# A fused retention and feed-forward kernel: turning the normalized rows of the last stage on VectorE and by transfers, with the up projection six blocks ahead

## What is computed

```python
def _moe2_ref(x, w_in, w_out, g_ln):            # x: 3072 x 512, w_in: 512 x 1024, w_out: 1024 x 512
    h = x @ w_in
    h_max = np.max(h, axis=-1, keepdims=True)
    e = np.exp(h - h_max)
    sm = e / (np.sum(e, axis=-1, keepdims=True) + 1e-09)
    solu = h * sm
    mu = np.mean(solu, axis=-1, keepdims=True)
    var = np.mean((solu - mu) ** 2, axis=-1, keepdims=True)
    ln = (solu - mu) / np.sqrt(var + 1e-06) * g_ln
    return (ln @ w_out).astype(np.float32)
```

## Time and profile before

| | us |
|---|---|
| median of three runs | 980.58 (980.35 to 981.1) |
| profiled execution | 983.99 |
| its span, first to last instruction | 982.2 |
| TensorE busy | 958.3 (98%) |
| VectorE busy | 616.8 (63%) |
| ScalarE busy | 548.3 (56%) |
| GpSimd busy | 135.5 (14%) |

### The profile page before, as it was taken

How to read it: one execution, slowest core, us unless ns; L and a number is a source line. 1 busy time by engine, 2 the same in 40 slices (tenths; PEclk the granted TensorE clock), 3 DMA queues, 4 the chain that set the end, 5 groups by cost and what they waited for, 6 DMA issues and landing times.

```text
span 982.2 us, 15207 instructions
## 1 busy us (share of the span) xinstructions
PE 958.3 (98%) x5494; PEld 849.6 (86%) x5494; DVE 616.8 (63%) x1054; ACT 548.3 (56%) x940; POOL 135.5 (14%) x170
## 2 busy tenths in 40 slices
PE   8879899999999999999999999999999999999998
PEld 4666787887899999999999999999888888888887
DVE  3777886777778653544678877677554444544442
ACT  3554645555465442433445555554687776667765
POOL 4313401102015510000151101010000000000000
PEclk9989999999999999999999999999999999999999
DMA  8747636536143513131553735521411111111100
GB/s 264 226 138 213 185 134 184 171 141 185 54 182 113 193 49 114 65 113 57 174 200 117 242 116 179 178 81 43 161 44 43 43 43 43 43 43 43 46 29 33
DMA packets 82320, 116.03 MB, mean 118 GB/s; under 512 B 7120, under 2 KB 62800, under 8 KB 82256
## 3 DMA queue, kind: packets, MB, share of 16 engines
q1 hardware_dynamic: 76800, 98.79, 30.6%
q0 software_dynamic: 4736, 15.73, 4.6%
q10 hardware_dynamic: 720, 0.66, 0.2%
HBM read 77.41 MB, written 37.75 MB: 117 GB/s over the span
## 4 chain that ended last, share of the span: by engine, by line
PE 83%; DVE 5%; issue 3%; DMA 3%; ACT 2%; POOL 2%; SPq 1%; DVEq 0%; ACTq 0%; POOLq 0%
PE psum L884 10%; PE psum L887 10%; PE psum L886 10%; PE psum L359 9%; PE psum L361 9%; PE psum L360 9%; PE psum L922 6%; PE psum L920 6%; PE psum L923 6%; PE psum L777 3%; PE psum L811 2%; PE psum L964 2%; PE psum L801 2%; PE psum L790 2%; DMA w_raw<-weights 1%
## 5 line engine op out<-in xcount | busy, mean ns | idle before, releaser
L884 PE MATMUL psum<-xo_hi,w_hi 128*128 128x384 f32 x560 | 195.3, 349 | 6.7 <-DVE psum L1494 2.6
L887 PE MATMUL psum<-xo_hi,w_lo 128*128 128x384 f32 x560 | 188.4, 336 | 0.0
L886 PE MATMUL psum<-xo_lo,w_hi 128*128 128x384 f32 x560 | 188.3, 336 | 0.0
L884 PEld LDWEIGHTS psum<-xo_hi,w_hi 128*128 128x128 f32 x560 | 105.9, 189 | 13.1 <-DVE xo_lo L1480 3.8
L886 PEld LDWEIGHTS psum<-xo_lo,w_hi 128*128 128x128 f32 x560 | 105.9, 189 | 0.8 <-issue 0.3
L1102 ACT ACTIVATE xo_hi<-b 128x768 fp32r<-128x768 f32 x84 | 70.6, 846 | 63.6 <-PE psum L923 51.9
L887 PEld LDWEIGHTS psum<-xo_hi,w_lo 128*128 128x128 f32 x560 | 105.7, 189 | 0.0
L1374 DVE TENSOR_TENSOR xo_lo<-b,xo_hi 128x768 fp32r<-128x768 f32 x84 | 80.0, 955 | 34.3 <-ACT xo_hi L1102 34.0
L359 PE MATMUL psum<-w_in_hi,x_hi 128*128 128x512 f32 x192 | 76.8, 400 | 0.3 <-ACT h_buf L1223 0.3
L361 PE MATMUL psum<-w_in_hi,x_lo 128*128 128x512 f32 x192 | 74.9, 390 | 0.0
L360 PE MATMUL psum<-w_in_lo,x_hi 128*128 128x512 f32 x192 | 74.9, 390 | 0.0
(11 more groups left out here) (128 smaller groups left out, 2065.8 us busy)
## 6 DMA issues: line engine op xcount, KB each, us to landing
act_dram<-act_buf SPq DMA_DIRECT2D x48, 384.0 KB, 2.4
b<-act_dram SPq DMA_DIRECT2D x48, 384.0 KB, 4.8
kq_buf<-k_t SPq DMA_DIRECT2D x32, 192.0 KB, 2.7
kq_buf<-q_t SPq DMA_DIRECT2D x64, 96.0 KB, 3.0
q_dec<-q_t SPq DMA_DIRECT2D x32, 192.0 KB, 2.5
w_raw<-weights POOLq DMA_DIRECT2D x12, 512.0 KB, 4.6
x_dram<-x_tile SPq DMA_DIRECT2D x4, 1536.0 KB, 6.0
x_tile<-x_dram SPq DMA_DIRECT2D x4, 1536.0 KB, 6.8
```

The lines of the kernel that those rows point to most:

```text
L884: pe.matmul(dst, hi[:, cols], xo_hi[:, i, kc, :], start=i in (P1, P7) and kc == 0, stop=False, skip_group_check=True)
L886: pe.matmul(dst, hi[:, cols], xo_lo[:, i, kc, :], start=False, stop=False, skip_group_check=True)
L887: mm = pe.matmul(dst, lo[:, cols], xo_hi[:, i, kc, :], start=False, stop=kc == HK - 1, skip_group_check=True)
```

## The change

It touches the last stage alone.

- The first tile keeps the way of before, turns on TensorE included. From block (1,0) on TensorE turns nothing. Instead ScalarE squares solu with the negative mean as bias (`square_solu`) and takes the root for two blocks at once (`deviation_of_pair`); VectorE inverts two at once (`invert_pair`), normalizes (`normalize`, mean and inverse deviation in one instruction), and turns the rows in 32x32 squares (`turn_blocks`) into a buffer z.
- SP then moves the squares to their partitions (`move_turned`): 16 transfers a tile, each from 32 partitions to 32 partitions, 512-byte runs, 128 KB, four for each quarter of the tile. They wait for the last `turn_blocks` of the tile.
- A block of the down projection is now 32 consecutive tokens out of each of the four blocks of the tile, so that its output rows lie in four runs. The output isn't scaled any more, since the rows are normalized already. `ln_high` and `ln_low` read SBUF instead of PSUM.
- TensorE runs the up projection six blocks ahead of the down projection instead of two: in the first tile each step has two up projections, then one per block, and for the last six blocks none.
- The loop on the device is gone: all tiles are written out. There is one order for tiles 1 to 5.

The diff, cut to what sets the order. The moves and the rows of an output, on SP:

```diff
+            def move_turned(t):
+                for i in range(PARTS):
+                    sp.wait_ge(z_ready, BLOCKS * t)
+                    sp.wait_ge(ln_lo_ready, 2 * (BLOCKS * (t - 1) + i + 1))
+                    for f in range(PARTS):
+                        sp.dma_start(ln_t[32 * f:32 * f + 32, i, :, :],
+                                     z_of(t)[32 * i:32 * i + 32, :, f, :, :].rearrange("p k j c -> p k (j c)")).then_inc(
+                                         ln_t_moved[i], DMA)
...
+                if t == 0:
+                    rows = out[n * P:(n + 1) * P, :]
+                else:
+                    rows = out[bass.ds(t * TC, TC), :].rearrange("(b i c) d -> i b c d", b=BLOCKS, i=PARTS)[j]
```

SP in tiles 1 to 5:

```diff
+                if t + 2 < C_TILES:
+                    load_pair(t + 2)
+                store_out(t - 1, 3)
+                for j in range(3):
+                    store_out(t, j)
+                if t + 1 < C_TILES:
+                    move_turned(t + 1)
```

TensorE in the first tile from its second block on, and in tiles 1 to 5:

```diff
+                    for j in range(1, BLOCKS):
+                        turn(0, j)
+                        both_up((2 * j + 2) // BLOCKS, (2 * j + 2) % BLOCKS)
+                        both_down2(0, j)
+                        both_up((2 * j + 3) // BLOCKS, (2 * j + 3) % BLOCKS)
+                    return
                 for j in range(BLOCKS):
...
+                    if run_up_of(t, j):
+                        both_up(*run_up_of(t, j))
+                    both_down2(t, j)
```

ScalarE in tiles 1 to 5:

```diff
+                    if j > 0:
+                        scale_out(t, j - 1)
+                    elif t > 1:
                         scale_out(t - 1, 3)
                     ln_high(t, j, 0)
                     ln_high(t, j, 1)
+                    last_up = (t + 1, j + 1) if j < 3 else (t + 2, 0)
+                    if last_up[0] < C_TILES:
+                        square_solu(*last_up)
+                        if j % 2 == 0:
+                            deviation_of_pair(t + 1, j // 2)
+                    if run_up_of(t, j):
+                        copy_h(*run_up_of(t, j), 0)
+                        if j % 2 == 1 and t + 2 < C_TILES:
+                            x2_high(t + 2, j // 2)
+                        copy_h(*run_up_of(t, j), 1)
+                        exponent(*run_up_of(t, j))
```

VectorE, the two new steps, and tiles 1 to 5:

```diff
+            def normalize(t, j):
+                dve.wait_ge(pair_rstd_ready, 2 * (t - 1) + j // 2 + 1)
+                dve.tensor_scalar(solu[:, j % 2, :], solu[:, j % 2, :], mean[:, j:j + 1], rstd[:, j:j + 1], ALU.add,
+                                  ALU.mult).then_inc(normalized, 1)
+            def turn_blocks(t, j):
...
+                dve.transpose(z_of(t)[:, :, :, j, :].rearrange("p k f c -> p (k f) c"),
+                              solu[:, j % 2, :].rearrange("p (b r) -> p b r", r=32)).then_inc(z_ready, 1)
...
+                    both_low(t, j)
+                    if t + 1 < C_TILES:
+                        if j % 2 == 0:
+                            invert_pair(t + 1, j // 2)
+                        turn_up(t + 1, j)
+                    if run_up_of(t, j):
+                        row_max(*run_up_of(t, j))
+                        if j % 2 == 1 and t + 2 < C_TILES:
+                            x2_low(t + 2, j // 2)
+                        take_up(*run_up_of(t, j))
```

More of the change, by code:

```diff
@@ L336, in x_bank, with tiles, run_up_of, solu_of @@
             return SUM if n == 1 else PX
-        def loop(eng, n, step):
-            step(0, True, False)
-            with eng.Fori(1, n - 1) as i:
-                step(i, False, False)
-            step(n - 1, False, True)
-        def tiles(eng, step):
-            loop(eng, C_TILES, step)
+        def tiles(step):
+            for t in range(C_TILES):
+                step(t)
+        def run_up_of(t, j):
+            tile, block = (t + 1, j + 2) if j < 2 else (t + 2, j - 2)
+            return (tile, block) if tile < C_TILES else None
+        def solu_of(t, j):
+            return solu_0[:, j, :] if t == 0 else solu[:, j % 2, :]
+        def z_of(t):
+            return z1 if t % 2 else z0
         def windows(attention_step, point):
@@ L1027, in _ @@
+            tiles(stage_c)
         @block.scalar
@@ L1570, in softmax_h @@
                 dve.wait_ge(sum_inverted, n + 1)
-                dve.scalar_tensor_tensor(out=solu[:, j % 2, :], in0=h_buf[:, j % 2, :], scalar=e_inv[:, one],
+                if n == 0:
+                    for s in range(4):
+                        dve.wait_ge(x2_stored[s], DMA * 2 * B)
+                dve.scalar_tensor_tensor(out=solu_of(t, j), in0=h_buf[:, j % 2, :], scalar=e_inv[:, one],
                                          in1=e_buf[:, j % 2, :], op0=ALU.mult, op1=ALU.mult,
```

313 lines of the change are left out of this document (209 added, 104 removed).

## The result

The changed kernel takes **993.32 us** (median of 4 runs, 992.76 to 994.5) against 980.84 of the kernel before beside it: ratio 1.0125, 95% interval 1.0107 to 1.0143. Measured a second time it was 992.09 against 981.84, ratio 1.0096 (1.0070 to 1.0122). So the change costs 12.5 us by the first pair of medians and 10.3 by the second. The forecast was 985.0 with a range to 992.0: the sign was right, and the time lies outside the range.

What follows compares the result with a forecast made beforehand. TensorE's own work was taken to bound the third stage. The terms -17.4 + 14.1 + 1.3 + 5.3 + 1.1 gave +4.4 us, from a median of 980.58 to 985.0, range 978.5 to 992.

Steps and rivals of the forecast that it cites:

- turns leave TensorE, 20 blocks: Third stage after the first tile: TensorE loses the turns, 0.87 us a block over 20 blocks, -17.4 us.
- hand-overs in the tail: Last six blocks: TensorE waits while ScalarE puts output ahead of the high halves, 2.35 us each, +14.1 us.
- moves at (5,0): Block (5,0) in the tail: its moves land later than the hand-overs alone would allow, +1.3 us (0 to 5).
- first tile: First tile of the third stage: TensorE waits 2.9 and 2.2 us, +5.3 us with the restarts.
- rival (d): Tail: the granted clock falls where TensorE idles 2.3 of every 7.8 us; 6 us more, 991; chance 0.05.
- last store: Kernel's end: store in four runs of 32 rows, +2.2 us if on four DMA engines, else 0; +1.1 taken.
- What bounds the kernel: Third stage: it lasts as long as TensorE's own work; work leaving its queue comes off the end unless somebody becomes late.
- Steady tiles: Tiles 1 to 3: ScalarE about 7.5 and VectorE 7.1 us a block fit under TensorE's 10.90; the moves stay hidden.
- The tail's waits: Last six blocks: TensorE waits about 2.2 us for the low half five or six times, output ahead of high half.
- rival (a): First tile: its hand-over costs nothing and the last store is as before; -2.0 us, 978.6; chance 0.13.
- (e): Last store: dealt to four DMA engines, 2.2 us instead of 1.1, 986.1 in all; chance 0.3.
- Profiled execution and median: Whole kernel: profiled execution 983.99 us, median of the runs 980.58; differences were taken to carry over, giving 985.0.

Runs made afterwards that it cites:

- e5: Changed kernel plus nine extra 512-column products on TensorE ahead of each of the last six down projections: 987.17 us, ratio 1.0057.
- e7: Changed kernel with e1's order, last square and deviation also before output, two of (5,0)'s moves on ScalarE's queue, last store in four from two queues: 978.25 us.
- e8: e9 plus 14 extra 512-column products on TensorE ahead of the down projection of (5,0): 975.86 us, ratio 0.9938.
- e9: e7 with all four moves for block (5,0) issued by SyncE again: 977.38 us, ratio 0.9951.
- e4: Changed kernel with e1's order, last store as four transfers of 32 rows, and e3's earlier inverse together: 978.9 us, ratio 0.9965.
- e1: Changed kernel with ScalarE making the two high halves before scaling the previous block's output in the last six blocks: 981.4 us, ratio 0.9984.
- e3: Changed kernel with VectorE inverting the deviation of (0,3) before the turns of (1,2) and (1,3) in the first tile: 993.05 us, ratio 1.0101.

## Why the prediction was right in its sign and wrong in its size

Its sum, term by term, from the two traces of the changed kernel:

| step | forecast | measured |
|---|---|---|
| turns leave TensorE, 20 blocks | -17.4 | -17.8 (20 x (11.77 - 10.88)) |
| hand-overs in the tail | +14.1 | +13.4 (6 x 2.23) |
| moves at (5,0) | +1.3 | 0, hidden behind the half clock of (4,3); 1.1 in e5 |
| first tile | +5.3 | +4.7 to +4.9, what is left over of the chain |
| clock in the tail, rival (d) | 0 | +4.8 and +6.4 (3 and 4 stretches of 1.6) |
| last store | +1.1 | +3.8 |
| sum | +4.4 | +8.9 and +10.7 |

**What bounds the kernel: right.** TensorE's steady block fell to its 48 matmuls, and the 12 blocks between (1,1) and (4,1) took 130.56 us in nine of the twelve traces of this order. In e7, e8 and e9 it is 132.9, since there the output of (4,1) itself stands 2.4 us further back in ScalarE's queue; the eleven steps ahead of it are 10.88 as well.

**Steady tiles: right.** The 32x32 turn takes 1.246 us (1.2 forecast), normalization 0.81 (0.75), and VectorE 32.08 of 50 us, 7.0 a block (7.1). ScalarE was 7.0 (7.5). Sixteen moves are issued in 11 to 12 us (10) and in the steady tiles TensorE doesn't wait for them; the first quarter takes 5.8 us from its first issue to the start of the high half (e4), where I had 4.8 to its landing.

**The tail's waits: right** in place, number, releaser and size. e1 shows that the order of output and high half makes them.

**The first tile: near in its sum.** The two waits were forecast as 2.9 and 2.2 and are 2.3 and 1.5; in one trace the clock stood in for the second. The +4.7 to +4.9 is a remainder; the waits by themselves are 3.8 where 5.1 were forecast. e3 shows that the inverse behind the turns, which I held against rival (a), isn't the cause.

**The clock: the step that failed.** I weighed rival (d) with the slices of the page, in which TensorE is busy eight tenths at a clock of nine. A slice is 24.6 us long and says nothing of a stretch of 3 us behind a gap of 2. I also read slices one, two and five and passed over the third, the one nearest to the tail's share: TensorE is busy seven tenths there and the clock is at eight. The row that spoke for it, 0.83 in a window of 10 us with 8.40 us busy, was the nearest row by length, and the tail (5.8 of 8 us busy) lay below it. I gave the mechanism 6 us, near the 4.8 and 6.4 that it cost, but a chance of 0.05 and nothing in the sum. e5 settles the cause: fill the gap and it is gone.

**The last store: a term mis-sized.** The mechanism of (e) was right, and its price was 3.8 us, beyond my upper end of 2.2. The end counted the data at a quarter of the rate (3.0 us; the trace has 256 KB at up to 103 GB/s) and left out the 2 us at under 50 GB/s ahead of it. I also took the middle of two ends where a stated rule pointed to one.

**Profiled execution and median.** I carried the differences from an execution of 983.99 us over to a median of 980.58. The part ahead of the change varies by 3.5 us between executions (716.9 to 720.4), so the sum holds against a chain of the stage, not against one execution's time; this added up to 3.5 us of uncertainty that the range didn't have. It bears on the miss: with the chains' +8.9 and +10.7 on 980.58 the time would have been 989.5 and 991.3, inside the range with the clock and the store as wrong as they are; that would have been luck.

With (d) at its own price and the last store at the measured one the sum is 4.4 + 6 + 2.7 = 13.1, against +8.9 and +10.7 in the traces. 1.3 of the difference is the moves at (5,0), which are hidden, and 0.7 the hand-overs; the rest is the number of stretches.

## What to carry to other kernels

Where a pipeline drains, its hand-overs open up: price each at the sum of the operations between the last matmul and the next (here 2.2 us), and the stretch at the lower clock that can follow it (here 1.6 us) on top. If a gap can't be closed, cheap matmuls into a free bank keep the clock (5 us won here with 54 of them), and the next thing to look for is what the closed gaps had hidden (here the moves, 4.1 us). The last transfer of a kernel stands on the path with its full time: look at the outermost size of its pattern (here one transfer of 4 x 32 rows took 2.9 us longer to the end than four of 32 rows).

## What the runs showed of the hardware

- A hand-over in which TensorE waits 1.9 us can bring a stretch of matmuls at half the pace (0.43 in place of 0.227 us per 512 columns), eight of them or 1.6 us; it did behind three and four of six in the two traces of the changed kernel. Gaps of 1.0 us in e5, 1.5 in e8 and 0.3 in e1 brought none, and neither did one of 2.3 in the second trace of the changed kernel. Behind waits of 4.1 us 7 and 8 matmuls were slow, behind 4.5 and 4.8 us 14 and 13.
- A store of 256 KB as 4 x 32 rows x 512 takes 3.8 us longer to the end than one of 128 rows, at up to 103 GB/s with 0.19 to 0.29 of the engines busy; four transfers of 32 rows from one queue give back 2.9 us of it, from two queues 3.5.
- Moves of 32 partitions inside SBUF in runs of 512 bytes, sixteen in a row, go with 160 to 230 GB/s over all queues and eight to nine tenths of the engines busy.
- Two moves issued on ScalarE's queue took 3.11 us while SyncE issued others; two stores on it took 0.87 us. Sixteen moves on SyncE's queue alone took 11.1 to 12.9 us.
